# Sparse attention and two feed-forward layers on one core: the order of the short query blocks, and the joint between the layers

## The chip, the cores and the metric

The kernel runs on one core of a Trainium2 chip. The metric is the device time of one launch in microseconds (us), the median of several runs. PE is TensorE, DVE is VectorE, ACT is ScalarE, POOL is GpSimd, SP is the engine that here only issues DMAs.

## What is computed

Four batches of eight-head attention with 576 queries and keys each, head width 64, where every query keeps only its 32 largest scores; then two feed-forward layers over the 2304 rows of width 512 with a hidden width of 2048. All of it is float32; the kernel splits each operand of the big products into a high and a low part and sums three products.

```python
scores = scale * np.matmul(q, k.transpose(0, 1, 3, 2))
kth = np.partition(scores, -top_k, axis=-1)[..., -top_k:-top_k + 1]     # top_k = 32
scores = np.where(scores >= kth, scores, -1e9)
attn = softmax(scores); x = attn @ v                                     # rows: 4*576, width 8*64
h = x @ w_in;  g = h - np.tanh(h);                         x = g @ w_out
h = x @ w_in2; g = np.where(h > 0, h, np.exp(np.minimum(h, 0)) - 1); out = g @ w_out2
```

## The kernel before

**Units.** 576 queries are four full tiles of 128 and a tail of 64. A unit of attention is one tile and one head, or, for a tail, one pair of heads (two times 64 queries). `plan` (L36) lists them: 4 batches times (32 + 4) = 144 units. Each batch's four tail units stand behind its first tile: units 8 to 11, 44 to 47, 80 to 83 and 116 to 119. The tails of two batches make one tile of 128 rows, so there are 16 + 2 = 18 tiles of x.

**Slots.** Every engine but SP runs the same loop over slots s (L559 on PE, L676 on ACT, L796 on DVE, L898 on POOL); there is no barrier, only semaphores between the engines. A unit passes through the engines over some five slots: PE makes the scores of unit s+1, ACT copies them, DVE finds the 32 largest of unit s and s-1 (four MAX8, L764, and three MATCH_REPLACE8, L773, each over 128x576), POOL takes the biases, ACT cuts and exponentiates, DVE inverts the sum, POOL scales (`norm`, L881), PE turns unit s-3 (L453) and, at the end of each pair of heads, multiplies with v (`attend`, L468). ACT copies the result out (`copy_x`), and in the slot in which a tile of x is complete, four slots behind its last unit, ACT makes its high part and POOL its low part (`x_low_part`, L863).

**The first layer inside the slots.** Two tiles make a group; 9 groups times 16 chunks of the hidden width are 144 steps. In slot s PE does `h_step` (12 products with w_in, L489) for one chunk and `y_step` (6 products with w_out, L506) for the chunk of the slot before. Between the two stand ACT (tanh; high part of g), and for the subtraction and the low part POOL up to slot 146 and DVE afterwards. A group's first step comes at the earliest READY = 5 slots behind the last unit of its second tile, and at the earliest behind the group before it (L91). Before, the second tile is complete with unit 19, so the steps fill slots 24 to 167. From that slot on the groups follow one another without a gap, and the earliest slot of groups 1, 5 and 6 is the very slot at which they start.

**Weights.** SP loads w_in and w_out in eight parts in slots 2 to 16; ACT and POOL split two pieces a slot in slots 5 to 20 (POOL one slot later, L857).

**The end of the first layer.** `at_last(s)` counts slots from the start of the last group. At 0 SP loads the first 512 rows of the first layer's result (`load_rows`); at 2 to 5 PE turns them (`rows_turn`, L520), and in the same slot ACT takes the high part (L590) and DVE the low part (L738); at 6 to 9 the first parts of the second layer's weights are split (L744, L749). After the last slot PE has `h2(0, CPB, 0)` and `h2(0, CPB, 1)` (12 products each, L536), then the loop of `y2` (12 products, L553) and `h2`. Between an h2 and its y2 stand ACT `exp` (L717), DVE (L837, L840), ACT high part (`elu_hi`, L590) and POOL low part (`elu_lo`, L922). `elu_hi` shares its memory with `y_rows`, from which the first layer's last rows are saved, so the first `elu_hi` waits until those saves have landed (L720 to L722).

## Time and profile before

| | |
|---|---|
| median of 3 runs | 1205.89 us (1204.3 to 1206.2) |
| the profiled execution's own time | 1206.25 us |
| its span in the profile | 1204.4 us |
| PE busy | 1144.6 us (95%) |
| DVE busy | 847.1 us (70%) |
| ACT, POOL busy | 696.4 us (58%), 496.1 us (41%) |
| PE in the chain that ended last | 87% |

The profile's page gives the busy share of each engine, the granted TensorE clock in 40 slices, the chain of work that ended last, and the costliest groups of instructions. A matmul's end is modelled, so a PE that is shown busy all the time may still be paced by something; start times are what to compare. The run has four stages: attention alone (0 to 123 us, PE two thirds busy, DVE fully), attention with the first layer (123 to 722 us, PE and DVE both shown fully busy), the rest of the first layer (722 to 787 us), the second layer (787 us to the end).

### The profile page before, as it was taken

The page shows a single profiled execution, that of the slowest core. Times are in us where ns is not written, and L with a number is a line of the kernel's source. Part 1 is how long each engine was busy: PE and PEld are TensorE (multiplying, and loading weights), DVE is VectorE, ACT ScalarE, POOL GpSimd, SP SyncE. Part 2 cuts the span into 40 slices and gives each one's busy share as a digit, 9 for nine tenths or more (in the row PEclk, how much of TensorE's full clock was granted, in tenths as well). Part 3 has the DMA queues.
Part 4 walks back from the last instruction along what each step waited for, and adds up shares of the span by engine and source line. Part 5 has one row for each costly group of instructions (what it writes and reads, how often), then busy time and mean ns, then how long its engine had stood idle before and what let it go on. Part 6 is the DMA issues. An engine that isn't in the chain of part 4 may idle for free.

```text
span 1204.4 us, 21473 instructions
## 1 busy us (share of the span) xinstructions
PE 1144.6 (95%) x7448; PEld 914.5 (76%) x7448; DVE 847.1 (70%) x1831; ACT 696.4 (58%) x1627; POOL 496.1 (41%) x806
## 2 busy tenths in 40 slices
PE   3667899999999999999999999999999999999997
PEld 2444777777777777777777788878888888888886
DVE  7999999999999999999999963445422222222221
ACT  3887778788778787777877773434322222222221
POOL 1676555565555555555555550012222222222221
PEclk9766999999999999999999999999999999999999
DMA  5430111201012110020100002530020020010000
GB/s 167 130 119 23 44 34 44 62 15 32 17 34 70 39 32 15 15 59 22 30 21 15 23 1 88 175 122 1 1 70 1 1 70 1 1 53 1 1 35 18
DMA packets 50714, 51.19 MB, mean 42 GB/s; under 512 B 5040, under 2 KB 37808, under 8 KB 50608
## 3 DMA queue, kind: packets, MB, share of 16 engines
q1 hardware_dynamic: 50608, 49.83, 13.7%
q8 instruction: 60, 0.98, 0.3%
q14 instruction: 46, 0.38, 0.1%
HBM read 40.37 MB, written 9.44 MB: 41 GB/s over the span
## 4 chain that ended last, share of the span: by engine, by line
PE 87%; DVE 9%; issue 1%; ACT 1%; DMA 1%; POOL 0%; SPq 0%; POOLq 0%; DVEq 0%; ACTq 0%
PE ps L489 19%; PE ps L506 17%; PE ps L553 16%; PE ps L536 16%; PE ps L468 7%; PE ps L442 6%; PE ps L453 4%; DVE work L773 4%; DVE best L764 4%; PE ps L454 1%; PE ps L520 1%; PE ps L439 1%; DMA ffn_rows<-y_rows 0%; POOL elu_lo L922 0%; ACT yT_hi L590 0%
## 5 line engine op out<-in xcount | busy, mean ns | idle before, releaser
L764 DVE MAX8 best<-work 128x8 f32<-128x576 f32 x432 | 315.9, 765 | 0.1
L922 POOL TENSOR_TENSOR elu_lo<-elu_h,elu_hi 128x512 fp32r<-128x512 f32 x72 | 93.1, 1293 | 379.0 <-ACT elu_hi L590 379.0
L773 DVE MATCH_REPLACE8 work<-best,work 128x576 f32<-128x576 f32 x288 | 219.5, 762 | 0.0
L837 DVE TENSOR_SCALAR exp_h<-exp_h 128x512 f32<-128x512 f32 x72 | 30.8, 427 | 256.2 <-ACT exp_h L717 256.2
L489 PE MATMUL ps<-xT_hi,w_in_hi 128*128 128x256 f32 x576 | 175.7, 305 | 2.2 <-POOL xT_lo L863 2.2
L489 PE MATMUL ps<-xT_lo,w_in_hi 128*128 128x256 f32 x576 | 163.4, 284 | 0.0
L489 PE MATMUL ps<-xT_hi,w_in_lo 128*128 128x256 f32 x576 | 163.0, 283 | 0.0
L717 ACT ACTIVATE exp_h<-ps 128x512 f32<-128x512 f32 x72 | 43.0, 598 | 202.9 <-PE ps L536 202.9
L489 PEld LDWEIGHTS ps<-xT_hi,w_in_hi 128*128 128x128 f32 x576 | 109.6, 190 | 50.0 <-issue 46.6
L881 POOL TENSOR_SCALAR scores<-scores,bias_and_sums 128x576 f32<-128x576 f32 x144 | 107.7, 748 | 59.5 <-DVE bias_and_sums L780 56.7
L600 ACT ACTIVATE scores<-ps 128x576 f32<-128x576 f32 x144 | 93.4, 648 | 62.9 <-PE ps L442 56.0
L506 PE MATMUL ps<-w_out_hi,gT_hi 128*128 128x512 f32 x288 | 124.5, 432 | 1.7 <-DVE gT_lo L791 1.7
L468 PE MATMUL ps<-weights_T,v_rows 128*64 128x128 f32 (+1 forms) x1600 | 106.3, 284 | 14.3 <-issue 9.4
L468 PEld LDWEIGHTS ps<-weights_T,v_rows 128*64 128x64 f32 x1600 | 87.7, 147 | 42.2 <-issue 42.2
L536 PE MATMUL ps<-yT_hi,w_in_hi 128*128 128x512 f32 (+1 forms) x320 | 119.4, 373 | 0.0
L536 PE MATMUL ps<-yT_hi,w_in_lo 128*128 128x512 f32 (+1 forms) x320 | 119.2, 373 | 0.0
L536 PE MATMUL ps<-yT_lo,w_in_hi 128*128 128x512 f32 (+1 forms) x320 | 119.2, 373 | 0.0
L605 ACT ACTIVATE scores<-scores,bias_and_sums 128x576 f32<-128x576 f32 x144 | 112.6, 782 | 10.2 <-POOL bias_and_sums L869 10.2
L442 PE MATMUL ps<-kT_halves,qT_twice 64*128 64x288 f32 x512 | 106.8, 497 | 12.0 <-ACT scores L600 6.8
L869 POOL TENSOR_TENSOR bias_and_sums<-best 128x2 f32<-128x2 f32 x144 | 28.1, 195 | 217.9 <-DVE best L764 216.6
L553 PE MATMUL ps<-w_out_hi,elu_hi 128*128 128x512 f32 x288 | 114.7, 398 | 3.3 <-POOL elu_lo L922 3.3
L590 ACT ACTIVATE weights_T<-ps 128x512 f32<-128x512 f32 (+1 forms) x288 | 111.4, 443 | 8.7 <-PE ps L454 8.7
(67 smaller groups left out, 2601.8 us busy)
## 6 DMA issues: line engine op xcount, KB each, us to landing
qT_twice<-qT SPq DMA_DIRECT2D x128, 64.0 KB, 2.2
w_in_raw<-w_in SPq DMA_DIRECT2D x8, 1024.0 KB, 5.2
w_out_raw<-w_out SPq DMA_DIRECT2D x8, 1024.0 KB, 5.5
kT_halves<-kT SPq DMA_DIRECT2D x64, 72.0 KB, 2.3
ffn_rows<-y_rows SPq DMA_DIRECT2D x18, 256.0 KB, 2.9
v_rows<-v SPq DMA_DIRECT2D x16, 256.0 KB, 2.8
rows<-ffn_rows SPq DMA_DIRECT2D x4, 1024.0 KB, 6.2
out<-out_rows SPq DMA_DIRECT2D x16, 256.0 KB, 2.5
```

Of the source, the lines that this page charges most:

```text
L442: mm = pe.matmul(ps[:, half, 0:HALF], q[rows, n % QRING, place_ * P:(place_ + 1) * P], keys[rows, buf, u.head, :], start=True, stop=True)
L468: mm = pe.matmul(ps[half * D:(half + 1) * D, B_OUT, cols], vals[:, c, u.pair, half * D:(half + 1) * D], weights, start=(c == 0), stop=(c = ...
L489: mm = pe.matmul(ps[:, B_H + i % 2, 0:N], l[:, kc, fs], r[:, kc, ring:ring + N], start=(kc == 0 and n == 0), stop=(kc == KC - 1 and n == 2))
L506: mm = pe.matmul(ps[:, B_Y + j, :], l[:, i % 2, ts], r[:, f, :], start=(f == 0 and n == 0), stop=(f == FC - 1 and n == 2))
L536: mm = pe.matmul(ps[:, B_H + f % 2, j * n * P:(j + 1) * n * P], l[:, kc, cs], r[:, buf, kc, 0:n * P], start=(kc == 0 and i == 0), stop=(kc ...
L553: mm = pe.matmul(ps[:, t, :], l[:, f % 2, ts], r[:, c, :], start=(c == 0 and i == 0), stop=(c == FC - 1 and i == 2))
L590: return nc.scalar.activation(out_, in_, ACT.Copy)
L600: nc.scalar.activation(sc[:, u.t % SCORES, :].rearrange("p (a s) -> p a s", a=2), ps[:, 0:2, 0:HALF], ACT.Copy, scale=SCALE).then_inc(copi ...
L605: nc.scalar.activation(sc[:, u.t % SCORES, :], sc[:, u.t % SCORES, :], ACT.Prelu, bias=bias[u.t % 2][:, 0:1], scale=1.0, alpha=STEEP).then ...
L764: nc.vector.max(best[:, u.t % 3, 1 + n * EIGHT:1 + (n + 1) * EIGHT], src).then_inc(done, 1)
L773: nc.vector.match_replace(wk[:, u.t % 2, :], best[:, u.t % 3, 1 + n * EIGHT:1 + (n + 1) * EIGHT], src, LOWEST).then_inc(chain if n < 2 els ...
L881: nc.gpsimd.tensor_scalar(w, w, rinv[u.t % 2], 1.0, ALU.mult, ALU.mult).then_inc(normed, 1)
```

## The change

Four edits, which belong together.

1. `plan`: the tails stand behind all tiles of batches 0 and 2, and ahead of the tiles of batches 1 and 3. Units 32 to 39 are the tails of batches 0 and 1, units 104 to 111 those of 2 and 3. The loads of k and v take their slots from the last use of each head (`last_use`).
2. With that the second tile is complete with unit 15, and the first layer's steps fill slots 20 to 163. Every group now starts in the very slot at which its second tile allows it. The last slot is 164, where it was 169.
3. ACT's and DVE's part of the turned rows is done one slot later than PE's (`at_last(s - 1) in ROWS_AT`), and rows, w_in and w_out of the second layer all stand one slot later from the last group's start (`ROWS_AT`, `w2_in_at`, `w2_out_at`).
4. `h2(0, CPB, 0)` is issued ahead of the last `y_step`. `elu_hi` and `elu_lo` get memory of their own, so their wait on the saves is gone; the two copies of the last y rows move on ACT from ahead of the first `exp` to behind the first `elu_hi`, and SP's save of them behind the loop.

```diff
 for b in range(batches):
+        if b % 2 == 1:
+            tails(b)
         for r in range(per):
             for h in range(heads):
                 units.append(Unit(len(units), b, b * per + r, head=h, pair=h // 2))
-            if r == 0:
-                for p in range(heads // 2):
-                    units.append(Unit(len(units), b, None, pair=p))
+        if b % 2 == 0:
+            tails(b)
...
-    LAST = y_slot[-1] + 1
+    LAST = y_slot[-1]
...
-        first = 24 if b == 1 else last_unit_of[(b - 1) * PER - 1] + 4
+        first = 16 if b == 1 else last_use[b - 2, H - 1] + 1
...
-            v_load_slot[first + 2 * j + 6] = (b, j)
+            v_load_slot[last_use[b - 1, 2 * j + 1] + 4] = (b, j)
...
-        w2_in_at = {6: (0, 1), 7: (2, 3)}
-        w2_out_at = {8: (0, 1), 9: (2, 3)}
+        w2_in_at = {7: (0, 1), 8: (2, 3)}
+        w2_out_at = {9: (0, 1), 10: (2, 3)}
-        ROWS_AT = {2: 0, 3: 1, 4: 2, 5: 3}
+        ROWS_AT = {3: 0, 4: 1, 5: 2, 6: 3}
...
+            load_w2_out(FB - 1)
+            for j in range(GN):
+                save_y(GROUPS - 1, j)
...
-                    pe.wait_ge(g_done_late, CHUNKS - EARLY)
+                    pe.wait_ge(g_done_late, CHUNKS - EARLY - 1 + f)
...
+                if s == LAST:
+                    h2(0, CPB, 0)
                 if s in y_in:
                     y_step(y_in[s])
...
-            h2(0, CPB, 0)
             h2(0, CPB, 1)
...
-                if at_last(s) in ROWS_AT:
-                    rows_high(0, ROWS_AT[at_last(s)])
+                if at_last(s - 1) in ROWS_AT:
+                    rows_high(0, ROWS_AT[at_last(s - 1)])
...
+                    high(g2_hi[:, f % 2, :], g2[:, f % 2, :]).then_inc(g2_high, 1)
                     if g == 0 and f == 0:
-                        for n in range(RING):
-                            sc_e.wait_ge(y_saved[n], (TILES - n + RING - 1) // RING * DMA)
-                    high(g2_hi[:, f % 2, :], g2[:, f % 2, :]).then_inc(g2_high, 1)
+                        for j in range(GN):
+                            copy_y(GROUPS - 1, j)
```

**Where the first layer begins, on POOL.** Before, the slots 22 to 24 around the low part of the second tile (xT_lo), with the last split of the weights two slots behind them:

```order
79 L857 TENSOR_TENSOR w_out_lo<-w_out_raw,w_out_hi 128x512 x2
80 L876 TENSOR_SCALAR bias_and_sums<-bias_and_sums 128x1
81 L869 TENSOR_TENSOR bias_and_sums<-best 128x2
...
92 L863 TENSOR_TENSOR xT_lo<-tile_xT,xT_hi 128x4x128
93 L881 TENSOR_SCALAR scores<-scores,bias_and_sums 128x576
94 L876 TENSOR_SCALAR bias_and_sums<-bias_and_sums 128x1
95 L869 TENSOR_TENSOR bias_and_sums<-best 128x2
96 L885 TENSOR_TENSOR gT_raw<-gT_raw,tanh_h 128x256
97 L881 TENSOR_SCALAR scores<-scores,bias_and_sums 128x576
98 L890 TENSOR_TENSOR gT_lo<-gT_raw,gT_hi 128x256
```

After, the same engine in slots 19 to 21:

```order
78 L877 TENSOR_TENSOR xT_lo<-tile_xT,xT_hi 128x4x128
79 L895 TENSOR_SCALAR scores<-scores,bias_and_sums 128x576
80 L871 TENSOR_TENSOR w_out_lo<-w_out_raw,w_out_hi 128x512 x2
81 L890 TENSOR_SCALAR bias_and_sums<-bias_and_sums 128x1
82 L883 TENSOR_TENSOR bias_and_sums<-best 128x2
83 L899 TENSOR_TENSOR gT_raw<-gT_raw,tanh_h 128x256
84 L895 TENSOR_SCALAR scores<-scores,bias_and_sums 128x576
85 L871 TENSOR_TENSOR w_out_lo<-w_out_raw,w_out_hi 128x512
86 L904 TENSOR_TENSOR gT_lo<-gT_raw,gT_hi 128x256
87 L871 TENSOR_TENSOR w_out_lo<-w_out_raw,w_out_hi 128x512
```

Two slots of split weights (four pieces) now stand behind xT_lo, and the last two pieces share a slot with the first layer's first subtraction and low part.

**Turned rows, on ACT.** Before, around the first two turned blocks (yT_hi), between the high part of g (gT_hi) of one slot and the tanh of the next:

```order
1225 L646 ACTIVATE tanh_h<-ps 128x256
1226 L590 ACTIVATE yT_hi<-ps 128x4x128
1227 L590 ACTIVATE gT_hi<-gT_raw 128x256
1228 L646 ACTIVATE tanh_h<-ps 128x256
1229 L590 ACTIVATE yT_hi<-ps 128x4x128
```

After, in the last turned slot:

```order
1242 L660 ACTIVATE tanh_h<-ps 128x256
1243 L604 ACTIVATE yT_hi<-ps 128x4x128
1244 L604 ACTIVATE w_in_hi<-w_in_raw 128x512 x2
1245 L604 ACTIVATE gT_hi<-gT_raw 128x256
1246 L660 ACTIVATE tanh_h<-ps 128x256
```

The order on the engine reads the same, but the block that yT_hi takes is now the one that PE turned in the slot before; the last of the four stands in the slot of the first pieces of w_in.

**The joint, on ACT.** Before, from the last high part of g to the second `exp`:

```order
1260 L590 ACTIVATE gT_hi<-gT_raw 128x256
1261 L590 ACTIVATE y_rows<-ps 128x4x128 x2
1262 L717 ACTIVATE exp_h<-ps 128x512
1263 L590 ACTIVATE elu_hi<-elu_h 128x512
1264 L590 ACTIVATE w_in_hi<-w_in_raw 128x512 x2
1265 L717 ACTIVATE exp_h<-ps 128x512
```

After:

```order
1264 L604 ACTIVATE gT_hi<-gT_raw 128x256
1265 L731 ACTIVATE exp_h<-ps 128x512
1266 L604 ACTIVATE elu_hi<-elu_h 128x512
1267 L604 ACTIVATE y_rows<-ps 128x4x128 x2
1268 L604 ACTIVATE w_in_hi<-w_in_raw 128x512 x2
1269 L731 ACTIVATE exp_h<-ps 128x512
```

The two copies of y rows have moved from ahead of the first `exp` to ahead of the second.

## Rows read from the trace of the kernel before

**Rows 1.** Busy time by stretch: stretch, length, engines busy (instructions), PEclk, DMA.

```profile
90.00:120.00 30.00, 21.48 (x122) 13.90 (x121) 30.00 (x69) 22.61 (x48) 19.43 (x29) 0.67 0.09 23
150.00:200.00 50.00, 50.00 (x383) 39.86 (x382) 50.00 (x114) 38.99 (x100) 26.97 (x51) 1.00 0.15 41
```

**Rows 2.** DVE in order of time: start, length, line; units 20 and 143 begin.

```profile
102.94 0.76 DVE L764 MAX8 best<-scores 128x8 f32<-128x576 f32 x1
...
703.42 0.80 DVE L764 MAX8 best<-scores 128x8 f32<-128x576 f32 x1
```

**Rows 3.** Chain of waits, h_step of slot 134: start, length, what.

```profile
661.46 1.63 PE ps L489 x12
```

**Rows 4.** Chain of waits, behind attention: one slot's h_step and y_step.

```profile
730.29 1.43 PE ps L489 x12
731.72 1.39 PE ps L506 x6
```

**Rows 5.** ACT's copy of unit 143's scores, in order of time.

```profile
700.81 0.64 ACT L600 ACTIVATE scores<-ps 128x576 f32<-128x576 f32 x1
```

**Rows 6.** PE and POOL in order of time, slots 20 to 25.

```profile
120.40 0.76 PE L442 MATMUL ps<-kT_halves,qT_twice 64*128 64x288 f32 x4
...
133.45 0.76 PE L442 MATMUL ps<-kT_halves,qT_twice 64*128 64x288 f32 x4
...
104.57 2.51 POOL L857 TENSOR_TENSOR w_out_lo<-w_out_raw,w_out_hi 128x512 fp32r<-128x512 f32 x2
...
122.07 1.27 POOL L863 TENSOR_TENSOR xT_lo<-tile_xT,xT_hi 128x512 fp32r<-128x512 f32 x1
```

**Rows 7.** The first h_step: chain of waits, and the stretch 124 to 126 us.

```profile
123.39 2.93 PE ps L489 x12
...
124.00:126.00 2.00, 2.00 (x11) 2.00 (x11) 2.00 (x5) 0.36 (x1) 0.34 (x2) 0.50 0.33 86
```

**Rows 8.** Chain of waits, h_step of two slots that hold tail units.

```profile
242.01 1.63 PE ps L489 x12
246.99 1.63 PE ps L489 x12
```

**Rows 9.** Group 1's start in slot 40, POOL and PE in order of time.

```profile
200.18 1.29 POOL L863 TENSOR_TENSOR xT_lo<-tile_xT,xT_hi 128x512 fp32r<-128x512 f32 x1
...
202.40 0.39 PE L489 MATMUL ps<-xT_hi,w_in_hi 128*128 128x256 f32 x1
```

**Rows 10.** PE and DVE in order of time, slots with turned rows and behind.

```profile
741.40 0.28 PE L489 MATMUL ps<-xT_hi,w_in_hi 128*128 128x256 f32 x1
...
744.58 0.36 PE L489 MATMUL ps<-xT_hi,w_in_hi 128*128 128x256 f32 x1
...
746.57 0.50 PE L506 MATMUL ps<-w_out_hi,gT_hi 128*128 128x512 f32 x1 [0.32 <-DVE gT_lo L791]
...
758.75 1.29 DVE L744 TENSOR_TENSOR w_in_lo<-w_in_raw,w_in_hi 128x512 fp32r<-128x512 f32 x2
```

**Rows 11.** Chain of waits: h_step of slot 159.

```profile
759.76 1.44 PE ps L489 x12
```

**Rows 12.** The joint in the chain of waits: start, length, what.

```profile
788.71 4.43 DMA ffn_rows<-y_rows
...
795.31 4.62 PE ps L553 x12
799.93 2.79 PE ps L536 x12
802.72 2.72 PE ps L553 x12
```

**Rows 13.** The joint in order of time, PE and POOL.

```profile
784.96 0.39 PE L506 MATMUL ps<-w_out_hi,gT_lo 128*128 128x512 f32 x1
...
799.76 0.40 PE L536 MATMUL ps<-yT_hi,w_in_hi 128*128 128x512 f32 x1
...
805.29 1.30 POOL L922 TENSOR_TENSOR elu_lo<-elu_h,elu_hi 128x512 fp32r<-128x512 f32 x1 [5.79 <-ACT elu_hi L590]
```

More of the change, by code:

```diff
@@ L38, in plan, with tails @@
     units = []
+    def tails(b):
+        for p in range(heads // 2):
+            units.append(Unit(len(units), b, None, pair=p))
     for b in range(batches):
+        if b % 2 == 1:
+            tails(b)
         for r in range(per):
@@ L117, in build @@
         q_load_slot.setdefault(-2 if n < QRING else qgroups[n - QRING][-1].t, []).append(n)
+    last_use = {}
+    for u in units:
+        for h in (2 * u.pair, 2 * u.pair + 1) if u.tail else (u.head,):
+            last_use[u.batch, h] = u.t
     k_load_slot = {}
     for b in range(1, B):
-        first = 24 if b == 1 else last_unit_of[(b - 1) * PER - 1] + 4
+        first = 16 if b == 1 else last_use[b - 2, H - 1] + 1
         for h in range(H):
@@ L126, in build @@
     for b in range(1, B):
-        first = last_unit_of[b * PER - 1] - (H - 1)
         for j in range(PAIRS):
-            v_load_slot[first + 2 * j + 6] = (b, j)
+            v_load_slot[last_use[b - 1, 2 * j + 1] + 4] = (b, j)
     scratch = nc.dram_tensor("ffn1_rows", [TILES * P, DM], F32, kind="Internal").ap()
@@ L189, in build @@
         at[0] = xt_at
-        g2_hi = place("elu_hi", [P, 2, BANK], F32R)
-        g2_lo = place("elu_lo", [P, 2, BANK], F32R)
+        at[0] += KC * RING * P * 4
         e2 = place("exp_h", [P, 2, BANK])
@@ L199, in build @@
         res = place("out_rows", [P, CPB, DM])
+        g2_hi = place("elu_hi", [P, 2, BANK], F32R)
+        g2_lo = place("elu_lo", [P, 2, BANK], F32R)
         assert at[0] <= attention_end
@@ L319, in load_k @@
                 if b > 1:
-                    sp.wait_ge(scored, last_unit_of[(b - 1) * PER - 1] - (H - 1) + h + 1)
+                    sp.wait_ge(scored, last_use[b - 2, h] + 1)
                 for half in (0, 1):
@@ L326, in load_v @@
                 if b > 0:
-                    sp.wait_ge(attended, event_of[last_unit_of[b * PER - 1] - (H - 1) + 2 * j + 1] + 1)
+                    sp.wait_ge(attended, event_of[last_use[b - 1, 2 * j + 1]] + 1)
                 sp.dma_start(vals[:, 0:FULL, j, :], v[b][j, 0:FULL * P, :].rearrange("(c p) d -> p c d", p=P)
@@ L817, in _ @@
                     difference(h_in[s])
-                if at_last(s) in ROWS_AT:
-                    rows_low(0, ROWS_AT[at_last(s)])
+                if at_last(s - 1) in ROWS_AT:
+                    rows_low(0, ROWS_AT[at_last(s - 1)])
                 for n in w2_in_at.get(at_last(s), ()):
```

## The prediction

> **What bounds the kernel now.** I read the busy time by stretch first. In 90 to 120 us DVE is busy all the time, PE for 21.48 of 30 us at a granted clock of 0.67; in 150 to 200 us both are shown busy all the time and the clock is 1.00 [rows 1]. Since a PE that is shown busy may still be paced by another engine, I then took start times. DVE begins unit 20 at 102.94 and unit 143 at 703.42 [rows 2]: 600.48 / 123 = 4.882 us a unit, with or without the first layer beside it. PE begins the h_step of slot 40 at 202.40 [rows 9] and that of slot 134 at 661.46 [rows 3]: 459.06 / 94 = 4.884 us a slot. So as long as attention runs, a slot costs some 4.88 us, whatever of the first layer stands in it, and PE has just enough time for a whole step of it. Once attention is over, a slot is one h_step and one y_step with nothing else, 1.43 us to the next start and 1.39 [rows 4]: 2.82 us, bound by PE alone. What is to be seen is the exchange: a step that moves from behind attention into it saves 2.82 us and costs nearly nothing, as long as PE was idle there. Slots 20 to 23 are such slots (PE two thirds busy).
>
> The first step was not free: PE made the scores of slot 24 at 120.40 and those of slot 26 at 133.45 [rows 6], 13.05 us for two slots instead of 9.77. PE lost 3.3 us against DVE there. POOL's xT_lo ended at 123.34 [rows 6], and the h_step behind it took 2.93 us instead of 1.63, at a granted clock of 0.50 [rows 7]. This lag stayed to the end of attention, and DVE did not feel it: ACT's copy of unit 143's scores ended at 701.45 [rows 5], 1.97 us before DVE began with them.
>
> **The change, part by part.** The sum is made against the profiled execution's own 1206.25 us, which is 0.36 over the median.
>
> *Four steps earlier.* The steps fill slots 20 to 163. Attention still has 144 units and ends where it ended; behind its last turned unit (slot 146) stand 17 steps instead of 21. Four slots of 2.82 go: **-11.3**. It needs every group to be in time, for now all nine start in the earliest slot possible. Before, three of them did, and one shows the margin: in slot 40 xT_lo ended at 201.47 and PE began at 202.40 [rows 9], 0.9 us to spare. The last group starts in slot 148, behind a slot of 2.82 us instead of 4.88: the copy of the last attend, ACT's high part and POOL's low part (1.27 [rows 6]) have to fit into that slot. I add 0, with up to 1 us if they don't.
>
> *The start among the splits.* The lag of 3.3 us now arises in slots 20 to 22, and there the splits of w_out still run. Two of them take POOL 2.51 us [rows 6]; beside attention and the first layer together POOL was busy 26.97 of 50 us [rows 1], 2.6 us a slot, so it has some 5.1 us to do in slot 21 against a slot of 4.88. xT_lo itself stands ahead of them and waits for the same DVE result as before. I take +0.3 us. Bounds: -1.3, if the clock happens to be full for the first h_step (2.93 against 1.63), and +4.9, one whole slot, if DVE is made to wait.
>
> *Tails.* Four of the 16 tail units had stood in slots in which PE had time; now all are beside the first layer. Two such slots are 4.98 us apart [rows 8], 0.10 more than 4.88. Four times that is 0.4; part of it the lighter slots take back: **+0.3**. Eight in a row push PE back by 0.8 us at most against a margin of 1.97, so DVE should not wait. The loads of v for batch 1 can start only when the tails of batch 0 have been multiplied, in slots 35 to 38, and are wanted in slots 39 to 42. Three slots (14.6 us) cover them, behind them on SP's queue stand loads of q and k that are wanted as late; costed at nothing. If the cover failed, PE would wait, up to four times.
>
> *Turned rows a slot later.* Before, PE's turned block comes last in its slot, ACT and DVE handle it there, and the low part of g for the next y_step stands behind it on DVE; PE waited for just that [rows 10]. From h_step 154 at 741.40 [rows 10] to h_step 159 at 759.76 [rows 11] it is 18.36 us. The one undisturbed slot with a turned block took 3.18 (741.40 to 744.58). Four of these and one plain one are 15.54, so 2.8 us were lost. With the handling one slot later the block is there when ACT and DVE come to it and all of it fits under the next h_step: -2.8. But the fourth block now stands in one slot with the first two pieces of w_in, which take DVE 1.29 us [rows 10]; with the 0.7 us of the block that slot is late by about 0.7. Net **-2.1** (from -2.8 to -1).
>
> *The joint.* PE began the last product of the last y_step but one at 784.96, and the h2 behind the first y2 at 799.76 [rows 13]; the first of these takes some 0.23 more to the next start (1.39 / 6 [rows 4]), so 14.57 us lie between. In it are one y_step (1.39), two h2 (2.79 each) and one y2 (2.72) [rows 4, 12], 9.7 us of work. The rest are the wait of the last y_step for its low part, the wait for the saves (the DMA of 4.43 us is in the chain [rows 12]), and a y2 that took 4.62 us instead of 2.72 because the clock had fallen after that wait. After the change h2 covers the first wait, and the DMA is no longer in the way. Does the rest close? With h2's start as S, its low part is ready at S + 6.83 (h2 at 799.76, POOL's elu_lo to 806.59 [rows 13]), and PE has h2, y_step, h2 until S + 6.97. So it closes by a hair: **-4.8** (from -5 to -2.4: late by half a microsecond, and 1.9 more if the clock falls again). Behind it ACT has two copies of y rows more ahead of the second `exp`, about 1.1 us. The second y2 comes 5.5 us after the first, so that is hidden.
>
> The page "TensorE: Matmul & The Clock Gate" of the Trainium skill (part 1, the HAM clock gate) says that the clock is halved after PE has been idle and comes back once it is busy. The joint's rows agree (4.62 against 2.72 behind a wait), and by that rule the dip goes with the wait, which is what the sum says. The same rule speaks against an early start, since a PE that is often idle begins the layer at half clock; that would leave the sum as it is, for the row of slot 24 has it already.
>
> Sum: -11.3 + 0.3 + 0.3 - 2.1 - 4.8 = -17.6. 1206.25 - 17.6 = 1188.65, called **1188.6 us**. Everything behind the joint is unchanged.
>
> **The rivals.** *The joint stays open (1191).* The low part is late by half a microsecond and the clock falls again: 2.4 of the 4.8 us stay. For it: the margin is 0.14 us. Against it: all its pieces are measured in the steady loop, and the h2 between has no other wait.
>
> *The start collides (1193.5).* Splits, first step and xT_lo overload POOL and ACT in slots 20 to 22, DVE stands still once and the whole grid moves by a slot, 4.9 us. For it: 5.1 us of work in a slot of 4.88. Against: it is one slot, and before and behind it POOL has time (19.43 of 30 us busy [rows 1]).
>
> *More than the sum (1185).* The clock is full at the first step (-1.3), the shared slot costs nothing (-0.7), and about half of the 3.3 us of lag does not arise (-1.5), since PE's waits at slot 24 (xT_lo was its own) need not fall alike: 1188.6 - 3.5 = 1185.1. Nothing in the rows speaks for it but that a start can fall either way.
>
> *Slower (1218): the clock does not come up.* The mechanism: in slots 20 and following the granted clock is what it is in 90 to 120 us (0.67 and, in pieces, 0.50) and does not rise when the first layer begins. A slot full of PE work at half clock costs up to 4.9 us more. The point from which it decides is 17.6 / 4.9 = 3.6 slots; lasting six slots it gives 1206.25 - 17.6 + 29.4 = 1218. Against it: before, the clock was back after one h_step. By the skill's rule of the clock gate named above it should rise too.
>
> *The moved steps save nothing*, because PE is the bound in slots 20 to 23 too: 1206.25 - 6.3 = 1200. Against it stand PE's 21.48 us in 30, at a reduced clock at that.
>
> **How the numbers follow.** Forecast 0.70, joint open 0.08, collision 0.08, more 0.06, nothing saved 0.04, slower 0.03; 0.01 is left for the unforeseen. The forecast's own range is 1186.5 to 1191. The range takes in the two rivals above it and the one below: 1185 to 1194. About 0.2% (2.4 us) is what a measurement of this kernel can tell from no change; faster by more than that 0.96, within it 0.01, slower 0.03.
>
> **What would show it.** First h_step some 19.5 us earlier, near 104 us, and DVE's units still 4.88 us apart, unit 143 near 703.4; last attend near 721; then slots of 2.82 with 3.2 to 3.3 in the four turned ones and one of about 3.5 behind them. The chain of waits without a DMA at the joint, and the first y2 at 2.7 to 2.8 us. From the h2 behind the first y2 to the end of the span 404.6 us as before. It is wrong if DVE shows idle time in attention, if PE waits for xT_lo at a group's start or for v at slots 39 to 42, or if the clock's row shows new dips.

## The result, and the profile after

| | before | after |
|---|---|---|
| median of four runs | 1205.10 us (1203.67 to 1206.20) | 1192.95 us (1191.20 to 1194.66) |
| ratio to before, 95% interval | | 0.990 (0.9876 to 0.9923) |
| profiled execution | 1206.25 us | 1194.63 us, span 1192.8 |

The kernel is 12 us faster where 17.6 were forecast: inside the wide range (1185 to 1194), but 4.35 us above the forecast and outside the forecast's own range (1186.5 to 1191). The profiled executions are 11.6 us apart. Three points of each chain of waits cut them into four stretches: the `h_step` of slot 147 (the first with nothing of attention beside it), the start of the joint, and the `h2` behind the first `y2`. The joint starts in before 0.23 behind the last start of rows 13's first product (785.19), in after with the first `h2` (775.24).

| stretch | before | after | difference | forecast |
|---|---|---|---|---|
| start to slot 147 | 721.63 | 724.55 | +2.92 | +0.6 |
| slot 147 to the joint | 63.56 | 50.69 | -12.87 | -13.4 |
| the joint | 14.74 | 9.80 | -4.94 | -4.8 |
| behind the joint, to the end of the span | 404.47 | 407.76 | +3.29 | 0 |

The two gains are there nearly in full. Two losses of some 3 us each, of which one was not in the sum and the other was in its bounds only, stand against them. Two rows of before, in its chain (start, length, what): slot 147, and a `y2` of the second layer's steady loop, to which the part on the joint comes back.

```profile
721.63 1.63 PE ps L489 x12
...
808.25 2.75 PE ps L553 x12
```

In after L502 is `h_step`, L519 `y_step`, L533 the turning of a block of rows, L549 `h2`, L566 `y2`, L455 the scores, L481 the attend.

**The start.** Chain of waits of after, slots 20 to 22, and two stretches of it (busy time by engine, then PE's granted clock):

```profile
104.03 2.93 PE ps L502 x12
...
108.93 2.40 PE ps L481 x20
...
112.59 2.11 PE ps L502 x12
```

```profile
104.00:106.00 2.00, 1.97 (x9) 1.97 (x10) 2.00 (x6) 1.50 (x4) 2.00 (x3) 0.50 0.28 69
...
112.00:114.00 2.00, 2.00 (x12) 1.48 (x9) 1.46 (x4) 0.82 (x2) 1.27 (x3) 0.59 0.00 0
```

The first `h_step` begins at 104.03, as forecast, and takes the 2.93 us of [rows 7]. But PE's clock stays at 0.50, the lower level, until some 113 us: the attend takes 2.40 us (1.24 in the chain near 723) and the second `h_step` 2.11. DVE and PE in order of time, idle time and its releaser in brackets:

```profile
104.03 0.58 PE L502 MATMUL ps<-xT_hi,w_in_hi 128*128 128x256 f32 x1 [2.22 <-POOL xT_lo L877]
...
107.81 0.75 DVE L778 MAX8 best<-scores 128x8 f32<-128x576 f32 x1
113.32 0.76 DVE L778 MAX8 best<-scores 128x8 f32<-128x576 f32 x1 [0.55 <-ACT scores L614]
...
206.60 0.76 DVE L778 MAX8 best<-scores 128x8 f32<-128x576 f32 x1
211.58 0.76 DVE L778 MAX8 best<-scores 128x8 f32<-128x576 f32 x1
...
704.93 0.75 DVE L778 MAX8 best<-scores 128x8 f32<-128x576 f32 x1
```

DVE's units were 4.88 us apart to the end; here one takes 5.51, since ACT's copy of its scores came late, and the two behind it take 5.03 and 5.18, the last with one more such wait, of 0.21. Four more units, from 201.66 to 221.53, right behind the first eight tails, take 4.94 to 4.98 each. Unit 143 begins at 704.93 instead of 703.42 [rows 2]. 1.5 of the 2.9 us are therefore DVE's (1.1 at the start, 0.35 behind the tails), the rest is PE's lag behind it.

**The slots behind attention.** The chain of after, a turned slot, and the slot in which the fourth block meets the first pieces of w_in:

```profile
742.54 1.43 PE ps L502 x12
743.97 1.39 PE ps L519 x6
745.36 0.44 PE ps L533 x4
745.79 1.43 PE ps L502 x12
...
749.05 1.44 PE ps L502 x12
...
751.42 0.69 DVE yT_lo L752
752.11 0.69 DVE w_in_lo L758 x2
...
753.23 0.43 DVE gT_lo L805
...
753.70 1.67 PE ps L519 x6
755.37 1.44 PE ps L502 x12
```

A turned slot is 3.25 us (742.54 to 745.79), with no wait: 2.82 plus the 0.44 of the block. Two slots lie between 749.05 and 755.37, 6.32 us, 0.68 more than 5.64: that is the shared slot, where `gT_lo` stands behind `yT_lo` and w_in's low parts on DVE.

**The joint and behind it.** Chain of waits, and the first `elu_lo` on POOL:

```profile
775.24 2.80 PE ps L549 x12
778.04 1.39 PE ps L519 x6
779.43 2.81 PE ps L549 x12
782.24 2.80 PE ps L566 x12
785.04 2.79 PE ps L549 x12
```

```profile
780.61 1.30 POOL L936 TENSOR_TENSOR elu_lo<-elu_h,elu_hi 128x512 fp32r<-128x512 f32 x1 [53.70 <-ACT elu_hi L604]
```

In the joint's part of the chain stands neither a DMA nor another engine; `elu_lo` ends at 781.91, 6.67 us behind the start of the first `h2`, and PE is busy until 782.24. What is not as forecast is `y2`: 2.80 instead of 2.72 to 2.75, and not here alone. Groups of instructions of after, from 790 to 1190 us (busy us, mean ns of one, idle time before):

```profile
L549 PE MATMUL ps<-yT_hi,w_in_hi 128*128 128x512 f32 (+1 forms) x308 | 114.7, 372 | 0.0
L566 PE MATMUL ps<-w_out_hi,elu_hi 128*128 128x512 f32 x281 | 112.1, 399 | 1.1 <-POOL elu_lo L936 1.1
L566 PE MATMUL ps<-w_out_lo,elu_hi 128*128 128x512 f32 x281 | 111.1, 395 | 0.0
```

No engine is waited for. From the `h2` behind the first `y2` to the last one of 12 products (the last group's have 24, of 256 columns) lie 61 pairs of `h2` and `y2` in both, and 14 turned blocks of 0.44: (1144.57 - 799.93 - 6.16) / 61 = 5.549 us a pair before, (1132.64 - 785.04 - 6.16) / 61 = 5.597 after. This makes 2.96 us. From there to the end of the span it takes 60.16 instead of 59.83, since the last group's pairs take 5.64 instead of 5.61: 0.33 more, together the tail's 3.29.

### The profile page after: what moved, and what is told of

It reads as the page before. It is cut to its first block, busy times and chain, and to the rows that moved or that the text cites. A ratio compares the mean times of both kernels' runs of the same rounds, so it can differ in the third digit from the quotient of the medians.

```text
span 1192.8 us, 21470 instructions
## 1 busy us (share of the span) xinstructions
PE 1143.2 (96%) x7448; PEld 912.6 (77%) x7448; DVE 843.8 (71%) x1823; ACT 695.3 (58%) x1631; POOL 505.6 (42%) x814
## 4 chain that ended last, share of the span: by engine, by line
PE 90%; DVE 7%; issue 1%; POOL 1%; ACT 0%; DMA 0%; SPq 0%; POOLq 0%; DVEq 0%
PE ps L502 19%; PE ps L519 17%; PE ps L549 17%; PE ps L566 16%; PE ps L481 7%; PE ps L455 6%; PE ps L466 5%; DVE work L787 4%; DVE best L778 3%; PE ps L467 1%; PE ps L452 1%; PE ps L533 1%; POOL w_in_lo L871 0%; DMA kT_halves<-kT 0%; POOLq L142 0%
## 5 line engine op out<-in xcount | busy, mean ns | idle before, releaser
L778 DVE MAX8 best<-work 128x8 f32<-128x576 f32 x432 | 309.5, 743 | 0.1
L787 DVE MATCH_REPLACE8 work<-best,work 128x576 f32<-128x576 f32 x288 | 213.0, 740 | 0.0
L502 PE MATMUL ps<-xT_hi,w_in_hi 128*128 128x256 f32 x576 | 176.4, 306 | 2.2 <-POOL xT_lo L877 2.2
L899 POOL TENSOR_TENSOR gT_raw<-gT_raw,tanh_h 128x256 f32<-128x256 f32 x127 | 94.1, 741 | 167.7 <-ACT tanh_h L660 167.7
L502 PE MATMUL ps<-xT_lo,w_in_hi 128*128 128x256 f32 x576 | 163.6, 284 | 0.0
L502 PE MATMUL ps<-xT_hi,w_in_lo 128*128 128x256 f32 x576 | 163.2, 283 | 0.0
L502 PEld LDWEIGHTS ps<-xT_hi,w_in_hi 128*128 128x128 f32 x576 | 109.9, 191 | 52.0 <-issue 48.7
L519 PE MATMUL ps<-w_out_hi,gT_hi 128*128 128x512 f32 x288 | 124.3, 431 | 0.4 <-DVE gT_lo L805 0.4
L549 PE MATMUL ps<-yT_hi,w_in_hi 128*128 128x512 f32 (+1 forms) x320 | 119.4, 373 | 0.0
L549 PE MATMUL ps<-yT_lo,w_in_hi 128*128 128x512 f32 (+1 forms) x320 | 119.3, 373 | 0.0
L549 PE MATMUL ps<-yT_hi,w_in_lo 128*128 128x512 f32 (+1 forms) x320 | 119.3, 373 | 0.0
L455 PE MATMUL ps<-kT_halves,qT_twice 64*128 64x288 f32 x512 | 106.7, 496 | 12.2 <-ACT scores L614 7.0
L481 PEld LDWEIGHTS ps<-weights_T,v_rows 128*64 128x64 f32 x1600 | 87.7, 146 | 38.1 <-issue 38.1
L566 PE MATMUL ps<-w_out_hi,elu_hi 128*128 128x512 f32 x288 | 114.9, 399 | 1.1 <-POOL elu_lo L936 1.1
L481 PE MATMUL ps<-weights_T,v_rows 128*64 128x128 f32 (+1 forms) x1600 | 106.5, 284 | 9.4 <-issue 8.4
```

The lines of the kernel that those rows point to most:

```text
L455: mm = pe.matmul(ps[:, half, 0:HALF], q[rows, n % QRING, place_ * P:(place_ + 1) * P], keys[rows, buf, u.head, :], start=True, stop=True)
L481: mm = pe.matmul(ps[half * D:(half + 1) * D, B_OUT, cols], vals[:, c, u.pair, half * D:(half + 1) * D], weights, start=(c == 0), stop=(c = ...
L502: mm = pe.matmul(ps[:, B_H + i % 2, 0:N], l[:, kc, fs], r[:, kc, ring:ring + N], start=(kc == 0 and n == 0), stop=(kc == KC - 1 and n == 2))
L519: mm = pe.matmul(ps[:, B_Y + j, :], l[:, i % 2, ts], r[:, f, :], start=(f == 0 and n == 0), stop=(f == FC - 1 and n == 2))
L549: mm = pe.matmul(ps[:, B_H + f % 2, j * n * P:(j + 1) * n * P], l[:, kc, cs], r[:, buf, kc, 0:n * P], start=(kc == 0 and i == 0), stop=(kc ...
L566: mm = pe.matmul(ps[:, t, :], l[:, f % 2, ts], r[:, c, :], start=(c == 0 and i == 0), stop=(c == FC - 1 and i == 2))
```

## Experiments

Before, run beside them, took 1204.28 to 1206.07 us in the median, and 1203.35 to 1206.48 in its single executions: it spreads by 3 us as well, and the one profile of it (1206.25) lies at the upper end. In the text below, S is the start of the first `h2` in the chain, and the tail is what lies behind the joint.

### What makes y2 slower, and the start later

`elu_hi` and `elu_lo` had stood in the first half of x's memory (xT_hi's, which `y_rows` shares), with `exp_h` and `elu_h` behind them in xT_lo's; edit 4 put them at the end of the second layer's part of attention's memory. The first run puts them into xT_lo's part of x's memory, 8 KB behind their old place, and sends the other two to the end:

```
-        e2 = place("exp_h", [P, 2, BANK])
-        g2 = place("elu_h", [P, 2, BANK])
+        g2_hi = place("elu_hi", [P, 2, BANK], F32R)
+        g2_lo = place("elu_lo", [P, 2, BANK], F32R)
...
-        g2_hi = place("elu_hi", [P, 2, BANK], F32R)
-        g2_lo = place("elu_lo", [P, 2, BANK], F32R)
+        e2 = place("exp_h", [P, 2, BANK])
+        g2 = place("elu_h", [P, 2, BANK])
```

> The changed kernel with one difference: elu_hi and elu_lo take the 8 KB where the low parts of x lay, and exp_h and elu_h take the new place behind out_rows. Same instructions in the same order. Question: why a y2 takes 2.80 us in the changed kernel and 2.75 before. Theory A (the address of the stationary operand elu_hi/elu_lo decides): y2 goes back to 2.75 us, 64 of them with four row blocks, and the time falls by 3.3 us against the changed kernel, to about 1189.7 (median of the changed kernel 1192.95). Theory B (it comes from something else in the new stage, such as the neighbours on ACT and DVE): y2 stays at 2.80 and the time at 1193 within 1 us.

1188.79 us (1187.89 to 1189.00), ratio 0.9865 (0.985 to 0.988). Its chain:

```profile
782.61 2.80 PE ps L549 x12
785.41 2.75 PE ps L566 x12
```

`y2` is back at 2.75, and from the `h2` behind the first `y2` to the end of the span it takes 404.59, as before. The place of the two buffers is the whole loss of the tail. `exp_h` and `elu_h`, which PE does not read, stand at the end of the area now and cost nothing. Slot 147 is at 722.23.

For the start two runs. In the first the splits of the weights begin a slot earlier:

```
-        W_FROM = 5
+        W_FROM = 4
```

> The changed kernel with the weights split one slot earlier (slots 4 to 19 on ACT instead of 5 to 20), so that ACT and POOL have no split beside the first layer's first steps. Theory A (the longer start, 15.5 us for two slots instead of 13.05, comes from the splits on ACT and POOL): DVE's wait of 0.55 us at unit 22 goes and the time falls by 1 to 2.5 us to 1190.5 to 1192. Theory B (it comes from the TensorE clock, which stays at half for 8 us): the slots 20 and 21 stay as long as they are and the time stays at 1193 within 1 us.

1191.81 us (1191.19, 1191.40, 1192.22, 1194.42). In its profiled execution (1191.40) the clock is at full right behind the first products, and slot 147 is at 721.31, 3.2 us earlier than in after:

```profile
104.00:106.00 2.00, 1.89 (x16) 1.89 (x17) 2.00 (x6) 1.93 (x5) 2.00 (x4) 1.00 0.29 77
```

But one of the four executions still took 1194.42, and the profiled executions of three runs below in which the splits stand as in after (`h2` behind, 721.15; `elu` first, 721.34; yT last, 721.28) had the clock at full from 104 us on as well. Less work on POOL in slots 20 to 22 does not decide it.

In the second PE has six products of 512 columns in slots 19 and 20 each, whose result nobody reads, ahead of the step:

```
+                if s in (h_slot[0] - 1, h_slot[0]):
+                    wait_w1("in", 0)
+                    for _ in range(6):
+                        pe.matmul(ps[:, B_Y, :], win_hi[:, 0, 0:P], win_hi[:, 0, 0:BANK], start=True, stop=True)
```

> The changed kernel with six extra products of 512 columns on PE in each of the slots 19 and 20, ahead of the first h_step, into a bank that is overwritten later: they fill PE's idle time and change nothing of the result. Theory A (the clock is what makes the start long, and it is low because PE had been idle): the first h_step runs at a clock nearer to 1.00 (1.6 to 2 us instead of 2.9), two slots from the scores of slot 20 take 11 to 13 us instead of 15.5, and the time falls by 2 to 4 us, to 1189 to 1191. Theory B (the splits on POOL and ACT make it long): no gain, or up to 2 us more, 1193 to 1195.

1192.12 us in the median of three (1191.50, 1192.12, 1192.22); a fourth took 2213.54, which nothing here explains; it is left out. Its clock and DVE's unit 143:

```profile
104.00:106.00 2.00, 2.00 (x15) 1.82 (x14) 2.00 (x6) 1.97 (x5) 2.00 (x3) 1.00 0.26 73
...
703.36 0.77 DVE L782 MAX8 best<-scores 128x8 f32<-128x576 f32 x1
```

At full clock DVE has no wait in attention, and keeps its 4.88 us a unit: (703.36 - 102.90) / 123 = 4.882. Slot 147 is at 721.44. The warm products buy no more than what an execution with a full clock has anyway. I had expected 1189 to 1191; the pace of DVE is the floor.

The same kernel as after, unchanged, once more:

> The changed kernel itself, unaltered, for the spread of its time. Its four runs so far lie at 1191.2 and at 1194.65, with nothing between. Theory A (the TensorE clock comes up at one of two moments at the start of the first layer): the runs again fall into two groups 3 to 3.5 us apart, and a profiled run of the lower group reaches the slot behind attention (slot 147) at 721.2 to 722.3, where the first trace had 724.55. Theory B (a spread of another kind): values between the groups.

1192.16 us (1191.23, 1192.11, 1192.22, 1192.39). Its profiled execution (1192.22) has the clock at 0.60 and 0.54 from 104 to 108 us and at 1.00 from then on, and slot 147 at 722.14:

```profile
106.00:108.00 2.00, 1.76 (x9) 1.35 (x7) 2.00 (x5) 0.97 (x4) 1.83 (x4) 0.54 0.32 80
108.00:110.00 2.00, 1.34 (x22) 1.20 (x22) 2.00 (x6) 2.00 (x5) 1.72 (x3) 1.00 0.13 37
```

Now the profiled executions can be laid beside one another: with the tail of after, the time less slot 147's start is 1194.63 - 724.55 = 470.08, 1192.22 - 722.14 = 470.08, 1191.40 - 721.31 = 470.09. **All of what differs between the two executions of this kernel, and the one with the earlier splits, arises ahead of slot 147**, and it goes with the clock of slots 20 to 22. The twelve profiled executions of versions that start in slot 20 fall into three groups by it: at full from 104 us on, slot 147 at 721.15 to 721.50 (six); back at full by about 108 us, 722.14 to 722.38 (four); back at about 113 us, 724.55 and 724.56 (two). In the last two the clock had still been at 1.00 in 100 to 102 us and had fallen while PE waited for xT_lo; in five of the first six (all but the one with the warm products) it was at 0.50 there and had come back by the first `h_step`. The four runs of after, two at 1191.2 and two at 1194.6, fit the two ends of it. So most of the 2.9 us of the first stretch belong to the execution that was profiled, and not to every one; how before's spread falls on its own stretches its one profile cannot say. What sets when the clock comes back these runs do not show.

### The four steps

Only the start of the first group is put back into slot 24, where it had been; everything else is as in after:

```
-        first = max(last_unit_of[tiles[g * GN + GN - 1]] + READY, h_slot[-1] + 1 if h_slot else 0)
+        first = 24 if g == 0 else max(last_unit_of[tiles[g * GN + GN - 1]] + READY, h_slot[-1] + 1 if h_slot else 0)
```

> The changed kernel with the first group held back to slot 24 as before (slots 24 to 167, last slot 168), all else as changed. It measures the four steps that start earlier. By the sum of the prediction (four slots of 2.82 us, less what the start costs more) the time rises by 11.3 less 2.4 to 2.9 for the longer start, to about 1193 + 8.6 = 1201.5. If the early start is worth the full 11.3, 1204; if the gain comes from the joint and the rows alone, it stays near 1193.

1202.55 us in the median of 11 (1202.47 to 1202.81), ratio to before 0.9981 (0.9972 to 0.9989). Slot 147 stays where it is and S moves:

```profile
721.15 1.63 PE ps L502 x12
...
783.10 2.80 PE ps L549 x12
```

S is at 783.10; in the run with the earlier splits, whose slot 147 is at 721.31, it is at 771.95. 11.15 us for four steps of 2.82, and 11.35 us against the runs of after at 1191.2. These 11 runs spread over 0.34 us only, but the late start alone does not do that: before starts in slot 24 too, and its 15 executions beside them spread over 3.13 us. Why is open. So ten of after's twelve microseconds hang on this one edit, and the rest of the change alone is worth 2 us against the runs of before beside it (3.7 against the profiled 1206.25), since a good part of the joint's gain is eaten by `y2`.

### Is it the address, and what about it?

Two other places in the same area: `elu` at its head, ahead of yT; and besides, yT at its end.

```
         at[0] = attention_at
+        g2_hi = place("elu_hi", [P, 2, BANK], F32R)
+        g2_lo = place("elu_lo", [P, 2, BANK], F32R)
         yt_hi = place("yT_hi", [P, 2, KC, BANK], F32R)
...
         res = place("out_rows", [P, CPB, DM])
-        g2_hi = place("elu_hi", [P, 2, BANK], F32R)
-        g2_lo = place("elu_lo", [P, 2, BANK], F32R)
```

> The changed kernel with elu_hi and elu_lo at the start of the second layer's area instead of at its end (48 KB lower, and yT, rows and out_rows 8 KB higher). Which address makes a y2 slow? Theory A1 (the high address of the stationary operand, above that of out_rows): y2 back at 2.75 us, h2 stays at 2.80. Theory A2 (any place that is not in the area of the first layer's x): y2 stays at 2.80.

```
         at[0] = attention_at
-        yt_hi = place("yT_hi", [P, 2, KC, BANK], F32R)
-        yt_lo = place("yT_lo", [P, 2, KC, BANK], F32R)
-        rows2 = place("rows", [P, CPB, DM])
-        res = place("out_rows", [P, CPB, DM])
         g2_hi = place("elu_hi", [P, 2, BANK], F32R)
         g2_lo = place("elu_lo", [P, 2, BANK], F32R)
+        rows2 = place("rows", [P, CPB, DM])
+        res = place("out_rows", [P, CPB, DM])
+        yt_hi = place("yT_hi", [P, 2, KC, BANK], F32R)
+        yt_lo = place("yT_lo", [P, 2, KC, BANK], F32R)
```

> The changed kernel with elu_hi and elu_lo first, then rows and out_rows, then yT_hi and yT_lo at the end of the area, so that the moving operand of h2 lies where elu_hi lay. Theory A1 (the high address of an operand slows PE, moving or stationary): h2 takes longer than 2.80 us, or one of its two buffers does, and y2 2.75. Theory A2 (only the stationary operand's place matters): h2 stays at 2.80 in all blocks.

One execution each: 1191.45 and 1191.37 us, `h2` and `y2` both 2.80, 407.83 and 407.79 behind the joint. The chain of the first:

```profile
787.37 2.80 PE ps L549 x12
790.17 2.80 PE ps L566 x12
```

So it is neither a high address nor the distance to the other operand: anywhere in this area `y2` takes 2.80. What the places in the area have in common is the remainder of their address by 128. Buffers are rounded up to 32 bytes in each partition. All up to `gT` are whole multiples of 128; `best` (99 numbers, 396 bytes, 416 with the rounding) and `small` (40 bytes, 64) follow, and 480 is 96 beyond a multiple of 128. There attention's memory begins, and each buffer in it is again a multiple of 128 long. x's memory begins at a multiple of 128. (All this is counted from the start of the kernel's memory, which is taken to be such a multiple itself; no trace shows it. The two runs that round the address, below, do not depend on it.) yT has stood at the remainder 96 in the kernel before too, and there `h2` took 2.79 to 2.80 [rows 12]. The next run moves the area to the next multiple of 128 and nothing else:

```
+        at[0] = (at[0] + 127) // 128 * 128
         attention_at = at[0]
```

> The changed kernel with one added line: the area of attention and of the second layer begins at a multiple of 128 bytes. Until now it began at a multiple of 32 that is no multiple of 64 (96 bytes over one of 128); w_in, w_out, the area of x and the high and low parts of g begin at multiples of 128. In the runs so far y2 took 2.75 us where elu_hi and elu_lo lay in the area of x and 2.80 wherever they lay in the other area, and h2 took 2.80 with yT in the other area at three offsets. Theory A (an operand of PE that begins 32 bytes off costs some 4 ns a product): y2 takes 2.75, and h2, whose moving operand yT is then aligned for the first time, 2.75 too: the end of the second layer shortens by 3.3 + 3.3 us, to about 1185.5. Theory B (it is the area, not the alignment): nothing moves, 1192 within 1 us. Theory C (only the stationary operand's alignment matters): y2 2.75, h2 2.80, about 1188.8.

1182.52 us (1182.04 to 1185.51), ratio 0.9811 (0.9798 to 0.9825): 10.4 us less than after in the median for one line, of which the tail has 9.2 and the rest is the start, with the clock at full in this profiled execution (slot 147 at 721.50). Chain of waits, and groups from 790 us on:

```profile
781.77 2.72 PE ps L550 x12
784.49 2.72 PE ps L567 x12
...
1125.82 2.87 PE ps L550 x24
```

```profile
L550 PE MATMUL ps<-yT_hi,w_in_hi 128*128 128x512 f32 (+1 forms) x304 | 111.4, 367 | 0.0
L567 PE MATMUL ps<-w_out_hi,elu_lo 128*128 128x512 f32 x280 | 109.1, 390 | 0.0
```

Both fall to 2.72. A pair takes (1120.38 - 781.77 - 6.16) / 61 = 5.450 us, 0.147 less than in after; the tail is 398.53 instead of 407.76. I had expected less (1185.5), as I had `y2` at 2.75 with its operand in place; with the neighbours in place too it is 2.72. In `h2` yT is the operand that moves through the array, in `y2` `elu` is the one loaded as weights; each costs when it is out of place. That holds for products of 512 columns only, as far as these runs go: the last group's `h2` of 24 products of 256 columns takes 2.87 with yT in place and 2.84 in after, and attention's products, whose operands were moved by the same line, keep their means between 300 and 700 us (the scores 455 ns of 288 columns, the attend 278 ns of 128). `h_step` and `y_step` are as before (1.63, 1.43, 1.39), and none of what they read was moved.

### The order at the joint

The first `h2` is put back behind the last `y_step`; the memory and ACT's order stay those of after:

```
-                if s == LAST:
-                    h2(0, CPB, 0)
                 if s in y_in:
                     y_step(y_in[s])
...
+            h2(0, CPB, 0)
             h2(0, CPB, 1)
```

> The changed kernel with h2(0, CPB, 0) back behind the last y_step, all else as changed (so elu_hi still does not wait for the saves). It splits the joint's 4.9 us. Expected from the rows: the last y_step waits 0.6 us for its low part as before, and y2 comes 6.83 + 0.15 us after the start of h2 while PE has only 5.6 us of work, so it waits 1.3 us: 1.9 us more between the last y_step but one and the second h2 (11.7 instead of 9.8), and 1.9 more again if the clock falls in that gap as it did before (13.6).

One execution: 1193.36 us. The chain from the last `h_step` on, and PE's granted clock while it waits for `elu_lo`:

```profile
769.03 1.45 PE ps L502 x12
...
771.82 0.44 DVE gT_lo L804
...
772.30 1.66 PE ps L519 x6
773.96 2.81 PE ps L549 x12
...
780.64 3.07 PE ps L566 x12
783.71 2.79 PE ps L549 x12
```

```profile
780.00:782.00 2.00, 1.36 (x6) 1.13 (x7) 1.23 (x3) 1.74 (x4) 0.59 (x1) 1.00 0.51 149
```

The last `y_step` waits for the low part, and `elu_lo` is late for `y2` as well, after which `y2` takes 3.07. Its last `h_step` starts at 769.03; one `h_step` and one `y_step` (2.82) later, at 771.86, S would be. From there to 783.71 is 11.85 us, against 9.80: **2.0 us for the order alone**, of the joint's 4.94. The other 2.9 are the copies and saves of the y rows ahead of `elu_hi`, and the dip of the clock behind that wait. Here PE idles for 1.08 us ahead of `y2` and the clock stays at 1.00 (in before it was at 0.50 from 796 to 798 us, behind an idle time of 2.22). The 3.07 is not the clock either: the first step behind a wait is shown 0.27 longer in the chain, `y_step` 1.66 instead of 1.39 and `y2` 3.07 instead of 2.80.

### Turned rows

ACT's and DVE's part is put back into the slot of PE's, and the area begins at a multiple of 64 that is none of 128, as a third point on the question above:

```
+        at[0] = (at[0] + 127) // 128 * 128 + 64
...
-                if at_last(s - 1) in ROWS_AT:
-                    rows_high(0, ROWS_AT[at_last(s - 1)])
+                if at_last(s) in ROWS_AT:
+                    rows_high(0, ROWS_AT[at_last(s)])
```

(and the same for DVE's `rows_low`)

> Two differences to the changed kernel, read in two stages that have nothing in common. First, ACT and DVE handle a turned block in the slot in which PE turned it, as before: the stretch from slot 147 to the first h2 is 50.7 us in the changed kernel; by the prediction's rows the four waits of 0.6 to 0.8 us come back (+2.8) and the shared slot's 1.0 goes, so 52.5. If the handling a slot later was worth nothing it stays at 50.7 or falls to 49.7. Second, the area of the second layer begins at a multiple of 64 bytes that is no multiple of 128: if 64 suffices, y2 (and h2, if the aligned run shows that too) takes 2.75 us, and 2.80 if it must be 128.

One execution: 1192.86 us. From slot 147 to S it is 722.35 to 774.79, 52.44 us, against 50.69. One of four equal slots:

```profile
740.49 0.45 PE ps L534 x4
...
740.96 0.61 ACT yT_hi L605
...
741.59 0.34 DVE yT_lo L753
...
742.20 0.42 DVE gT_lo L806
...
742.67 1.67 PE ps L520 x6
```

3.85 us a slot (742.67 to 746.52) instead of 3.25: 0.6 us four times, 2.4, of which the 0.68 of the shared slot, which is gone here, is given back.

The 64 gives a mixed answer: `y2` stays at 2.80, and `h2` is at 2.76 in the first row block and at 2.76 and 2.79 to 2.80 by turns behind it. The tail is 406.57, 1.2 less than in after, where the multiple of 128 gives 9.2. It helps the moving operand a little and the loaded one not at all. Remainders other than 0, 64 and 96 were not tried.

### The best of it

`elu` in x's memory, the earlier splits, and the pieces of the second layer's w_in and w_out a slot later, so that no slot is shared:

```
-        w2_in_at = {7: (0, 1), 8: (2, 3)}
-        w2_out_at = {9: (0, 1), 10: (2, 3)}
+        w2_in_at = {8: (0, 1), 9: (2, 3)}
+        w2_out_at = {10: (0, 1), 11: (2, 3)}
```

> The changed kernel with three differences: elu_hi and elu_lo in the old low parts of x (as in the placement run), weights split one slot earlier, and the first pieces of the second layer's weights one slot later (slots 8 to 11 from the last group's start instead of 7 to 10), so that no slot holds both a turned block and a piece of weight. Expected: placement alone 1188.8; the shared slot costs 0.8 to 1.0 us (slots 147 to 163 take 50.69 us, and 49.7 by the sum of their steps), so 1188.0; the earlier split nothing where the clock is up in time, since attention's end is then paced by DVE. If the later weights are missed by the first h2 or y2, 1189 or more.

1187.93 us (1187.31, 1187.49, 1188.38, 1190.77), ratio 0.987 (0.9855 to 0.9885). The profiled execution is the longest of the four, with the clock at half until past 112 us and slot 147 at 724.56. From slot 147 to S it takes 50.11, 0.6 less than in after.

With the area at a multiple of 128, and `elu` left in it:

> The changed kernel with the area aligned to 128 bytes, the weights split one slot earlier, and the second layer's first pieces one slot later. Expected by adding the single runs: if alignment gives what Theory A of the aligned run says, 1185.5 less 1.0 for the shared slot, 1184.5; by Theory C 1187.9 as the placed version with the same two edits. A run in which the clock comes up late at the first layer's start lies 3 us higher.

1181.53 us in the median of five (1181.38 to 1182.46), ratio 0.9799 (0.9786 to 0.9813), from slot 147 to S 50.12, `h2` and `y2` 2.72. It is 24.5 us faster than the kernel before, run beside it, and 11.4 faster than after.

## Where the prediction was right and where it was not

**The number: inside the range by luck.** The measured 1192.95 lies above the forecast's own range. The wide range holds it because it takes in two rivals, the open joint (1191) and the collision at the start (1193.5). The joint did close, POOL's load did not decide the start, and the largest part of the miss, in `y2`, is in no rival.

**DVE as the bound of attention: right.** Units 4.88 us apart, except where PE had fallen behind, and all nine groups in time; PE waits for xT_lo once, at the very first step, as in before, and never for v. One sign of being wrong did come, DVE's idle time in attention (0.55 and 0.21); it belongs to the start.

**Four steps earlier, -11.3: right.** 11.15 to 11.35 with only this undone.

**The start among the splits, +0.3, and tails, +0.3: mis-sized.** In the profiled execution the two together came to +2.92 and in that of the first version under "The best of it" to +2.93; in the ten other profiled executions that start in slot 20 they came to between -0.5 and +0.75, all against before's one 721.63. The step that failed is the choice of a value between the bounds: it took the lag from the rows of before, where the clock was back after one `h_step` [rows 7], as what the place costs. It is what one execution drew. The bound of +4.9 named the mechanism, DVE made to wait, and holds; the rival "the start collides" put it down to too much work for POOL and ACT, and that is not it, as POOL has the same work in the profiled executions of 1191.37 and 1191.45, whose clock was at full. It is the slower rival's clock, in a mild form: nine microseconds of half clock and 3 us lost instead of six slots and 29. The Trainium skill, page "TensorE: Matmul & The Clock Gate", Part 1, says that the number of slow products differs from run to run of one and the same kernel; the two profiled executions of after agree (the clock back at full by 108 us and at 113).

**"DVE should not wait" behind the tails: right only while PE's lag is small.** In after's profile four units behind the first eight tails take 4.94 to 4.98 us, 0.35 lost; where the clock was back by 108 us (the second profile of after) no unit is late.

**Turned rows, -2.1: a little too good, -1.6.** The waits removed are 2.4 and not 2.8: the sum took 3.18 for a turned slot from one interval of [rows 10], where it is 3.25. The shared slot costs 0.68, as in the sum; a `y_step` of 1.51 two slots on adds 0.1.

**The joint, -4.8: right (-4.94).** It closes, with 0.33 us to spare where 0.14 were forecast. Two of the 4.9 us come from the order, and 2.9 from the copies, the saves and the clock together.

**"Everything behind the joint is unchanged": wrong, +3.3.** This is the step that failed and that the sum had no bound for. The part on the change read "`elu_hi` and `elu_lo` get memory of their own" only as a wait removed. The address itself has a price of some 0.05 us for each of some 70 `y2`, and the kernel before had the like in `h2` all along, which no one could see, as all its `h2` of 512 columns were alike. Had the forecast left 3.3 us for it, it would have said 1191.9. Conversely, with the two buffers in x's memory the sum's own value comes out, 1188.79 against 1188.6; part of that is luck, as the sum starts from an execution at the upper end of before's spread, and against the runs beside it (1204.51) the gain is 15.7 and not 17.6.

## What to carry to other kernels

Work that moves under an engine that is the bound anyway is worth its full time at the end, and the steps can be counted from one row. When an edit moves a buffer that TensorE reads, note the remainder of its address before and after, and compare the mean length of that line's products in the two traces: here some 6 ns on each of more than 1400 products were worth 9 us, nearly as much as the four steps. And where a step begins on a PE that has been idle, one trace shows one draw of the clock; take the bound, or several executions.

## What was not expected of the hardware

- **The start address of an operand that TensorE reads.** Twelve products of 512 columns of fp32r take 2.80 us with the operand in question 96 bytes beyond a multiple of 128 in its partition and 2.72 with both lines' operands at a multiple, for the moving operand (`h2`) as for the loaded one (`y2`). At 64 beyond: 2.76 and 2.80 by turns moving, 2.80 loaded. The `h2` of 24 products of 256 columns gained nothing (2.87 at a multiple, 2.84 at 96 beyond). Aligning both was worth 9.2 us in the tail of 407.8. `y2` took 2.75 next to an `h2` whose operand was out of place, and 2.72 next to one in place, though its own operands were at multiples of 128 in both; why is open, and so is the mechanism.
- **The clock behind an idle PE** was back 4 us after the first product of the first `h_step` in one execution and 9 us after it in another, with the same instructions in the same order, and the whole kernel's time followed it, by 2.4 us between these two. An idle time of 1.08 us at the joint left it at 1.00.
